# An attention and mixture kernel: the expert weights laid on partitions in runs of consecutive rows

## The reference

```python
logits = x @ phi                        # 2304 x 32
d = softmax(logits, axis=0)             # over the tokens, for each slot
slot_input = (d.T @ x).reshape(E, S_per_e, D)
for e in range(E):
    h = np.maximum(slot_input[e] @ w1[e], 0.0)    # w1[e]: 512 x 1024
    slot_out[e] = h @ w2[e]                       # w2[e]: 1024 x 512
out = softmax(logits, axis=1) @ slot_out
```

## Time and profile before

| | us |
|---|---|
| median of 3 runs | 457.27 |
| the profiled execution | 456.89 |
| its span | 455.2 |
| TensorE busy (matmul) | 419.4 |
| VectorE busy | 233.8 |
| ScalarE busy | 212.5 |
| GpSimd busy | 70.9 |
| mean granted clock of TensorE | 0.976 |

### The profile page before, as it was taken

One profiled execution on the slowest core, in us unless ns is written; L12 is line 12 of the kernel. 1 busy time (PEld: TensorE's weight loads), 2 busy tenths in 40 slices (PEclk: granted clock), 3 DMA queues, 4 the chain that ended last, 5 costly groups with the idle time before them and its releaser, 6 DMA issues.

```text
span 455.2 us, 10183 instructions
## 1 busy us (share of the span) xinstructions
PE 419.4 (92%) x3764; PEld 341.4 (75%) x3764; DVE 233.8 (51%) x698; ACT 212.5 (47%) x601; POOL 70.9 (16%) x112
## 2 busy tenths in 40 slices
PE   3899999999999968896596999999999999999997
PEld 2788888878888844575465788888888888888885
DVE  2467686777677745040434554445444445444442
ACT  2788777777777600000615434433343433343431
POOL 1133133223223302000575200000000000000000
PEclk9999999999999987999897999999999999999999
DMA  9759989799898373999900010101010101010101
GB/s 176 192 147 259 238 241 233 232 219 255 214 278 239 110 275 119 386 385 396 374 8 1 1 46 1 46 0 46 0 46 0 46 0 46 0 46 0 46 1 48
DMA packets 75494, 61.41 MB, mean 135 GB/s; under 512 B 57792, under 2 KB 57792, under 8 KB 75456
## 3 DMA queue, kind: packets, MB, share of 16 engines
q1 hardware_dynamic: 75456, 60.89, 44.3%
HBM read 56.16 MB, written 4.72 MB: 134 GB/s over the span
## 4 chain that ended last, share of the span: by engine, by line
PE 85%; DVE 6%; ACT 4%; issue 3%; DMA 1%; SPq 0%; DVEq 0%; ACTq 0%
PE probs_turned L957 23%; PE out_turned L957 22%; PE scores L756 7%; PE probs_turned L765 4%; PE out_turned L781 4%; PE scores L939 4%; PE scores L885 4%; PE scores L900 3%; PE routes L811 3%; PE out_turned L785 3%; PE turns L739 2%; PE turns L796 2%; ACT probs L397 2%; PE turns L731 2%; PE routes L835 1%
## 5 line engine op out<-in xcount | busy, mean ns | idle before, releaser
L683 DVE SCALAR_TENSOR_TENSOR g<-u,scores 128x512 f32<-128x512 f32 x72 | 49.5, 688 | 110.5 <-ACT u L435 110.5
L440 ACT ACTIVATE g_hi<-g 128x512 fp32r<-128x512 f32 x72 | 45.5, 633 | 120.4 <-PE out_turned L957 120.2
L957 PE MATMUL probs_turned<-w_out_hi,g_hi 128*128 128x512 f32 x144 | 58.0, 403 | 7.3 <-DVE g_lo L689 3.9
L397 ACT ACTIVATE probs<-probs,rowmin 128x128 f32<-128x128 f32 (+1 forms) x160 | 62.0, 391 | 3.5 <-DVE rowmin L508 3.5
L957 PE MATMUL probs_turned<-w_out_lo,g_hi 128*128 128x512 f32 x144 | 57.8, 402 | 0.0
L957 PE MATMUL probs_turned<-w_out_hi,g_lo 128*128 128x512 f32 x144 | 57.0, 396 | 0.0
L957 PE MATMUL out_turned<-w_out_hi,g_hi 128*128 128x512 f32 x144 | 56.8, 394 | 0.0
L957 PE MATMUL out_turned<-w_out_lo,g_hi 128*128 128x512 f32 x144 | 56.7, 394 | 0.0
L957 PE MATMUL out_turned<-w_out_hi,g_lo 128*128 128x512 f32 x144 | 56.7, 393 | 0.0
L689 DVE TENSOR_TENSOR g_lo<-g,g_hi 128x512 fp32r<-128x512 f32 x72 | 53.4, 741 | 3.1 <-ACT g_hi L440 3.1
L756 PE MATMUL scores<-k_t,q_t 64*128 64x128 f32 (+2 forms) x576 | 42.7, 286 | 0.8 <-ACT k_t L375 0.8
(11 more groups left out here) (131 smaller groups left out, 626.9 us busy)
## 6 DMA issues: line engine op xcount, KB each, us to landing
weight_ring<-in_moe_w_dram SPq DMA_DIRECT2D x32, 1024.0 KB, 7.7
out_dram<-y SPq DMA_DIRECT2D x18, 256.0 KB, 2.0
q_in<-in_q_dram SPq DMA_DIRECT2D x16, 256.0 KB, 4.4
k_in<-in_k_dram SPq DMA_DIRECT2D x16, 256.0 KB, 4.8
v_in<-in_v_dram SPq DMA_DIRECT2D x16, 256.0 KB, 3.9
weight_ring<-in_moe_w_in_dram SPq DMA_DIRECT2D x8, 512.0 KB, 12.5
weight_ring<-in_moe_w_out_dram SPq DMA_DIRECT2D x4, 1024.0 KB, 15.3
q_in<-in_q_dram SPq DMA_DIRECT2D x4, 128.0 KB, 4.1
```

The costliest lines, as they stand in the source:

```text
L397: act.activation(probs[0:R, m % 2, h, :], probs[0:R, m % 2, h, :], ACT.Exp, bias=rowmin[0:R, m % 2, h:h + 1], scale=-1.0, accum_out=rsum[0 ...
L440: act.activation(g_hi[:, p % 2, :], g_sb[:, p % 4, :], ACT.Copy).then_inc(ghi_ready, 1)
L683: dve.scalar_tensor_tensor(out=g_sb[:, p % 4, :], in0=u_sb[:, p % 2, :], scalar=6.0, in1=bank[p % 4], op0=ALU.min, op1=ALU.mult).then_inc( ...
L957: ins = pe.matmul(bank[4 + kk][:, :], g[:, p % 2, cols], w[:, c, :], start=(p == 0 and i == 0 and a == 0), stop=(p == FPAIRS - 1 and i == ...
```

## The change

There are three edits. The view of a weight piece puts rows `4p` to `4p+3` of `w1` (rows `8p` to `8p+7` of `w2`) on partition `p`. A piece is then 16 KB of consecutive memory for each partition, and a half is 8 KB. Chunk `c` of `w1` now holds the rows `4p + c`, so chunk `c` of `x` has to hold the columns `4p + c`: `normalise` writes `x_held` with `c` as the fastest index of the output, four consecutive columns of `x` going to four places 516 bytes apart, while it reads PSUM in order. Chunk `c` of `w2` holds the rows `8p + c`, so the hidden columns have to come in that order: the `w1` product of quarter `j` reads the columns `8x + 2j + i`, for `i` 0 and 1 and `x` 0 to 127, two runs of 128 elements with a step of 8 elements (32 bytes). The number and size of the instructions and of the DMAs do not change.

```diff
         def piece(n):
             src = w1[n] if n < E else w2[n - E]
-            return src.rearrange("(c p) f -> p c f", p=P), ring[n % RING][:, :].rearrange(
+            return src.rearrange("(p c) f -> p c f", p=P), ring[n % RING][:, :].rearrange(
                 "p (c f) -> p c f", f=src.shape[1])
...
                 dve.wait_ge(o_turned, n + 1)
-                dve.tensor_tensor(x_held[0:R, n % XRING, :, 0:P].rearrange("p c (g d) -> p c g d", d=HD),
-                                  ps_a[0:R, :].rearrange("p (c g d) -> p c g d", g=2, d=HD),
-                                  rinv[0:R, 1, :].rearrange("p (c g) -> p c g", g=2).unsqueeze(3)
-                                  .broadcast_to([R, KC, 2, HD]), ALU.mult).then_inc(normed, 1)
+
+                dve.tensor_tensor(x_held[0:R, n % XRING, :, 0:P].rearrange("p c (h y) -> p h y c", h=HEADS),
+                                  ps_a[0:R, :].rearrange("p (h y c) -> p h y c", h=HEADS, c=KC),
+                                  rinv[0:R, 1, :].unsqueeze(2).unsqueeze(3)
+                                  .broadcast_to([R, HEADS, HD // KC, KC]), ALU.mult).then_inc(normed, 1)
...
                         ins = pe.matmul(bank[0][SLOTS * j:SLOTS * (j + 1), 0:CHUNK], slot_view[:, n, c, :],
-                                        w[:, c, j * CHUNK:(j + 1) * CHUNK], start=(n == 0 and c == 0),
+                                        w[:, c, :].rearrange("p (x a i) -> p a i x", i=2, a=QUADS)[:, j], start=(n == 0 and c == 0),
                                         stop=(n == E - 1 and c == KC - 1), tile_position=(0, SLOTS * j))
```

## The result

The changed kernel takes 474.07 us (median of 4 runs, 473.65 to 474.28), the kernel before 457.28 us beside it (456.95 to 457.64). The ratio is 1.0366, with a 95% interval of 1.035 to 1.0381: 16.8 us slower. The forecast was 456.9 us, and the range ended at 470.5. The time went the way of rival 1, and 5 us beyond its 468.9.

A forecast was written before the change was run, and what follows sets the result against it. TensorE was taken to bound the kernel, waiting for no weights during attention. Weight DMAs -0.4 us, `x_held` write 0 and `w1` read 0 summed to -0.4, so the median 457.27 becomes 456.9 us; range 453.9 to 470.5.

The forecast's parts named there:

- rival 1: `w1` products: the stepped read binds TensorE, 1.76 ns once per element, +12.6 us, about 1 back: 468.9 us; chance 0.26.
- What bounds the kernel: Whole kernel: TensorE, busy 419.4 of 455.2 us, sets the time; changing DMAs pays only where it waits for data.
- the four stops: TensorE among `w2` and first `w_in` products: 4.48 us of waits, read as program blocks fetched behind packets of data.
- Part 1: Weight loads: 2.56 us a MB, worth 0 by itself; shorter instruction-fetch waits give -0.4 us, ends 0 and -0.8.
- rival 3: Instruction fetches behind weight loads: queueing counted in packets, wait 3.7 us becomes 14, +9 us, 466.3 us; chance 0.07.
- rival 4: Instruction fetches behind weight loads: fewer packets let them through at once, three stops go, 3.6 us, 453.7 us; chance 0.12.
- The term of -0.4: Three instruction fetches behind weight pieces: waits shrink with the transfer rate; two thirds of -0.6 us taken.
- The sentence on the clock: TensorE's clock: said to go down in every longer pause, allowed for by half a us more on either side.
- Part 2: VectorE's write of `x_held`: 0 expected from elements 516 bytes apart, 691 ns kept; upper bound 1060 ns each.
- 4 x 0.37 = 1.5 us: Upper bound for the `x_held` write: +0.37 us at each of its four places on the chain, one per batch.
- The sign named for being wrong: Attention, up to 170 us: moving by more than 1.5 us would show the prediction wrong about what binds.
- Part 3: Stepped read of `w1` in its products: 0 expected, barely; 16.2 us at L885 would confirm it.

The follow-up runs named there:

- `w2` side alone: Kernel before, with only `w2` in the new layout and `w1` read with the 32-byte step; `x_held` write and `w1` layout old: 470.21 us, ratio 1.0261.
- the fifth kernel: Changed kernel, but `x_held` is written in order and the step is on the PSUM read; `w1` still read with the step: 471.07 us, ratio 1.0293.

## Why the prediction was wrong

**What bounds the kernel: right.** TensorE sets the time, and a faster transfer pays only where TensorE waits. The layout alone (ratio 1.0) and the version free of both costs (0.9991) show it, each with over 400 GB/s. The reading of the four stops as blocks of the program held up by data was right too, and the run with light loads shows it.

**Part 1, the DMAs: right in the sum, wrong in its sign.** I had 2.56 us a MB; in the changed kernel 8.45 MB go from 185 to 205 us, which is 2.48 a MB, a little faster than the 2.52 of my range's end. The wait of a fetch did not shrink with the rate. In the changed kernel it was 3.95 us (from 213.23 to the packet at 217.18) and 3.71 (from 219.67 to 223.38), against 3.8 and 3.7 before. But the 8 KB packets were through by then: all 719 and all 517 packets in these two stretches are under 8 KB. The fetch that did stand behind 8 KB packets is that of the layout alone, with 4.5 us. By packets, as rival 3 had it, it would have been 14, so that is out; rival 4, no wait, is out as well. The ground on which I had put both aside was thin, though. The packets of the earlier trace rows have 2.4 KB each by the mean and those of the earlier trace rows 2.6, so the two equal waits were not behind packets of one size and of twice that size. The term of -0.4 should have been 0. The sentence on the clock was wrong as well: it does not fall in every longer pause. Behind a stop of 2.5 us it was 1.00 in the kernel before and 0.71 in the changed one.

**Part 2, the write of `x_held`: the value was wrong and the bound of its length was right.** It took 1058 ns, and I had taken 0 "because the nearest rows for a write are writes". Those two writes, L618 and L662, went in runs of four elements and more, and told nothing of a write in which each element stands by itself; the reductions did, though they were reads. The bound for what of it reaches the path was wrong too: 4 x 0.37 = 1.5 us, where the `w1` products start 2.69 later. The last stretch shows part of it. The last write starts at 165.09 in place of 163.13; the first product behind it at 167.86 in place of 165.55, so 0.35 is added; the next ones run at a lower clock (0.47 and 0.63 us in place of 0.33 and 0.41), which makes the last 0.4. The other 1.96 us arise before it, and here the bound had counted the chain as it stood. In the changed kernel the chain runs through seven of the writes, not four. These three were not on it before:

```profile
44.22 1.04 DVE x_held L525
...
82.54 1.06 DVE x_held L525
...
121.12 1.06 DVE x_held L525
```

The write at 58.74 begins as early as before (58.75). The last writes of the next three batches begin 0.58, 1.18 and 1.96 us later than before, so 0.58, 0.60 and 0.78 are added in a batch, which is about two writes of 0.37 where the bound had one. So the write came to bind in places where 691 ns had been covered. This is read from the chain and the starts; no run parts the writes. VectorE's share of the chain went from 6 to 9%. The sign named for being wrong here, the attention's end moving by over 1.5 us, did come.

**Part 3, the read of `w1`: this is the step that failed.** I took 0, and the measured term is +13.5. The argument was that a record at L885 may use only half of what the port can give, since a step of the output layer reads an element in 0.45 ns. But a read with a step is another thing: 29.73 us / 64 / 256 = 1.81 ns an element for both passes together, where 0.83 was the limit for hiding it. That is VectorE's price (1.76) paid once, which is rival 1. (That an element is really fetched once, and not twice at half the price, is read from this equality and was not tested.) The run of the `w2` side alone has the same 29.8 us, and with the same columns read in pairs the products take 16.2 to 17.5. The port's rate in plain reads says nothing of its rate in reads with a step; the row that did was VectorE's, and beside it stood the rule of the Trainium skill. I had given both to the rival, with a chance of 0.26 where it should have been the forecast.

**Rival 1's 468.9 us** lacks 5.2. In the books of the profile: the products 0.9 longer (0.465 us a group in place of 0.451); part 2's 2.7, left out of the rival; 1.2 for the 1 us that was to come back from the stops and turned into 0.2 more (0.7 less of idle time, 1.4 more at the lower clock); and 1.0 behind L928, where I had nothing and which is no part of the change (see below). These sum to 5.8, in a profile that is 17.4 slower where the medians differ by 16.8. The range ended at 470.5, which is about rival 1 with part 2's bound of 1.5 on it. So it did put the two together, and still fell short: that bound was 1.2 too low, the products 0.9 too short, and the 1 us did not come back in this profile. It does where the clock holds: from the first `w2` product to that last step of the experts it is 26.0 us with the `w2` side alone and 26.3 in the fifth kernel, against 27.53 before.

**What stays open.** By ratios the two sides alone make 14.4 of 16.8 us, and 16.3 when counted against the 457.28 us beside the changed kernel, so how much is missing is within the noise of the medians. In the profiles the spans are 2.9 and 13.1 us longer than before, 16.0 together, against 17.4 of the changed kernel, and its 1.4 us of low-clock records are as large as the difference. Neither those nor the 1.0 us behind L928 belong to the change, by the other profiles. The low clock behind the third stop is seen in five of the profiles, one of them with the old layout. The stretch from L928 to the end is 237.8 to 237.9 us in five profiles, one with the old layout again, and 236.8 to 237.2 in the other seven, five with a new layout of `w1` among them. What decides the clock there is not shown.

## What to carry to other kernels

In these runs a float32 access that visits each 16 bytes of SBUF only once cost about 1.8 ns an element, whether TensorE read its moving side so or VectorE wrote so; two elements to 16 bytes were nearly free (9% on the product, nothing on the write). So if a layout needs a reordering, put its step on a read of PSUM by VectorE, or keep pairs together, before it goes into the moving read of a product. And look first for who waits for the transfer: here 8 KB stretches raised the rate by 8% and were worth nothing. A bound that counts how often an instruction stands on the chain holds only while the instruction keeps its length: a longer one can come onto the chain in more places, as the write did with seven for four.

## What the runs showed of the hardware that was not expected

- At 1.81 ns an element TensorE's granted clock made no difference. Two windows of the changed kernel, inside the `w1` products, as the earlier trace rows: 20 records in 2 us at a clock of 0.50, and as many at 0.98.

```profile
175.60:177.60 2.00, 2.00 (x20) 0.82 (x24) 1.20 (x2) 0.74 (x1) 0.61 (x1) 0.50 0.04 8
177.60:179.60 2.00, 2.00 (x20) 0.61 (x16) 1.86 (x5) 0.00 (x0) 0.00 (x0) 0.98 0.00 0
```

- One quarter of TensorE reading with a step of 32 bytes holds the other three, which read plainly, to its pace: 3.7 us a piece with one such quarter, 3.68 with four.
- VectorE's read of PSUM with a step of 16 bytes costs nothing (691 ns for 512 elements), its write to SBUF with the same step 0.8 ns an element more (1102 ns). The Trainium skill (PSUM — Partial Sum Buffer, Specifications) warns that a pattern with gaps in PSUM slows products; that is said of TensorE and was not tried here.
- The Trainium skill (Runtime: NRT & Kernel Launch, Instruction fetch mechanics) calls the cost of going from one block to the next mostly hidden. Not here: beside a full DMA queue it cost 5.9 us in 27.5.
- A memset by GpSimd and VectorE's scaling from SBUF to SBUF, 0.2 us apart in their starts, made the latter 2.08 us long in place of 0.31, in two profiles of eleven; in the other nine the starts lay as close together. What decides it is not shown.
